# The input rows of the expert tiles turned by the DMA in 16-bit halves instead of on TensorE

## The reference

```python
attn_out = attention(q, kv, w_sr)       # 2 x 12288 queries of 128, 768 pooled keys each
x = attn_out.reshape(24576, 128)
x = moe(x, w_gate, w1, w2)              # expert = argmax(x @ w_gate), 8 experts, F = 1024
                                        # out = gate * (relu(x @ w1[e]) @ w2[e])
x = moe2(x, w_gate, w_output_gate, w1, w2)   # the same, times sigmoid(x @ w_output_gate)[e]
```

## Time and profile before

| | us |
|---|---|
| median of 3 runs | 1875.81 (1872.98 to 1877.0) |
| profiled execution, span from first to last instruction | 2009.7 |
| PE busy | 1918.1 (95%) |
| PEld busy | 1879.5 (94%) |
| DVE busy | 1342.6 (67%) |
| ACT busy | 1054.8 (52%) |
| POOL busy | 739.4 (37%) |
| `turn_x` on PE (L1287), 400 transposes, busy | 76.3 |

### The profile page before, as it was taken

One profiled execution on the slowest core, in us unless ns is written; L12 is line 12 of the kernel. 1 busy time (PEld: TensorE's weight loads), 2 busy tenths in 40 slices (PEclk: granted clock), 3 DMA queues, 4 the chain that ended last, 5 costly groups with the idle time before them and its releaser, 6 DMA issues. The chain is left out here.

```text
span 2009.7 us, 53289 instructions
## 1 busy us (share of the span) xinstructions
PE 1918.1 (95%) x15716; PEld 1879.5 (94%) x15716; DVE 1342.6 (67%) x3525; ACT 1054.8 (52%) x2333; POOL 739.4 (37%) x823
## 2 busy tenths in 40 slices
PE   9999999999999999998999989899999999999998
PEld 7999999999999989898898889888999999999998
DVE  6788887888887666565566666666655555555555
ACT  3777777777776344344344444343444444444444
POOL 5456643466643323222222222222333333333333
PEclk8999999999999999999999999999999999999999
DMA  8355532355533211111321111142211114141111
GB/s 301 104 169 174 178 102 74 109 172 175 173 114 125 67 49 50 42 46 44 118 92 44 45 48 42 51 135 74 66 44 46 43 42 165 42 163 43 46 44 36
DMA packets 138040, 185.88 MB, mean 92 GB/s; under 512 B 17425, under 2 KB 95380, under 8 KB 134368
## 3 DMA queue, kind: packets, MB, share of 16 engines
q1 hardware_dynamic: 112640, 134.16, 20.9%
q0 software_dynamic: 25312, 50.65, 7.1%
HBM read 98.41 MB, written 87.63 MB: 93 GB/s over the span
## 5 line engine op out<-in xcount | busy, mean ns | idle before, releaser
L1718 DVE SCALAR_TENSOR_TENSOR h_lo<-psum,h_hi 128x512 fp32r<-128x512 f32 x800 | 541.2, 688 | 248.3 <-ACT h_hi L1509 198.4
L1509 ACT ACTIVATE h_hi<-psum 128x512 fp32r<-128x512 f32 x800 | 460.6, 598 | 259.1 <-PE psum L1303 244.9
L1303 PE MATMUL psum<-x_hi,w 128*128 128x256 f32 x1600 | 344.7, 290 | 66.6 <-DVE x_lo L1712 48.7
L413 POOL DMA_INDIRECT y_bucket<-kv_store,place x200 | 194.3, 971 | 542.1 <-DVE place L379 484.5
L1303 PE MATMUL psum<-x_hi,w_split 128*128 128x256 f32 x1600 | 339.6, 287 | 9.2 <-issue 2.8
L997 POOL DMA_INDIRECT out<-rows x200 | 193.9, 970 | 405.0 <-DVE rows L1738 368.5
L1303 PEld LDWEIGHTS psum<-x_hi,w 128*128 128x128 f32 x1600 | 270.2, 192 | 75.5 <-issue 55.2
L1320 PE MATMUL psum<-h_hi,w 128*128 128x256 f32 x1600 | 321.6, 285 | 0.7 <-DVE h_lo L1718 0.7
L413 POOL DMA_INDIRECT x_bucket<-rows,place x192 | 190.0, 990 | 293.2 <-DVE place L379 197.7
L1303 PEld LDWEIGHTS psum<-x_hi,w_split 128*128 128x128 f32 x1600 | 265.5, 189 | 17.4 <-issue 10.5
L1320 PEld LDWEIGHTS psum<-h_hi,w 128*128 128x128 f32 x1600 | 266.4, 195 | 1.3 <-DVE h_lo L1718 1.3
(11 more groups left out here) (177 smaller groups left out, 4385.1 us busy)
## 6 DMA issues: line engine op xcount, KB each, us to landing
w_table<-w_split SPq DMA_DIRECT2D x64, 512.0 KB, 3.5
w_raw<-in_moe_w SPq DMA_DIRECT2D x64, 256.0 KB, 4.1
xr<-x_bucket SPq DMA_DIRECT2D x100, 132.0 KB
xr<-y_bucket SPq DMA_DIRECT2D x100, 132.0 KB
kv_store<-in_kv SPq DMA_DIRECT2D x24, 512.0 KB, 9.3
q_in<-in_q SPq DMA_DIRECT2D x48, 256.0 KB, 2.7
w<-w_table SPq DMA_DIRECT2D x12, 1024.0 KB, 6.8
w_split<-w_table SPq DMA_DIRECT2D x8, 1024.0 KB
```

The lines of the kernel that those rows point to most:

```text
L413: nc.gpsimd.indirect_dma_start(r.bucket[:, :], bass.IndirectOffsetOnAxis(r.place[:, g, s:s + 1], 0), r.rows[:, g, s, LG:], None, bounds_ch ...
L1303: ins = nc.tensor.matmul(bank[p][:, m * BLOCK:(m + 1) * BLOCK], layer.w1[c % 2][:, hl, f], x[:, c % 2, :], start=k == 0, stop=k == 2)
L1509: nc.scalar.activation(h_hi[:, p, :], bank[p][:, :], ACT.Relu).then_inc(h_hi_done, 1)
L1718: nc.vector.scalar_tensor_tensor(h_lo[:, p, :], bank[p][:, :], 0.0, h_hi[:, p, :].bitcast(F32), ALU.max, ALU.subtract).then_inc(h_lo_done, 1)
```

## The change

Rows are stored in the tables with their 16-bit halves parted: 128 low halves, then 128 high halves. GpSimd does that in a new step `halve`, a copy of 128x512 elements of 16 bits for each half group (each block or tile), out of a new tile `pre_rows` (`pre_mid` in layer 1) into `rows`. `load_x` becomes two DMAs: a transposing one of 256 rows by 256 halves into `x_halves`, and a small one for `ID` and `GATE` into `tags`. VectorE gets a new step `join_x` at the front of each tile (ahead of `h_low` 0), a copy of 128x512 elements of 16 bits that puts the halves together again to float32 in `x_whole` (a part of `w_raw`). `x_high` and `x_low` read `x_whole` in SBUF instead of PSUM bank 5; `turn_x` is gone from TensorE. Row t of a tile is now token t of the load, where it was (2p + s); both sides of the row, the matmul and `tags`, follow that.

```diff
-PITCH = 132
+PITCH = 130
...
+        x_halves = sb("x_halves", [P, 4, 2, BLOCK], U16)
+        tags = sb("tags", [P, 4, SUB, PITCH - D], I32)
+        x_whole = w_raw[:, 0, 0:2 * BLOCK].rearrange("p (k t) -> p k t", k=2)
...
+        def halve(pool, r, i, gc):
+            if live(i, gc, r.groups, 2):
+                g = gc % 2
+                for h in range(2):
+                    at = slice(h * SUB, (h + 1) * SUB)
+                    wait(pool, r.row_step, i, UNROLL * r.row_steps, r.row_steps * (2 * gc + h + 1))
+                    pool.sem_inc(r.halve_go, 1)
+                    pool.tensor_copy(r.rows[:, g, at, 0:D].bitcast(U16).rearrange("p s (k d) -> p s k d", k=2),
+                                     r.pre[:, g, at, r.n * E:r.n * E + D].bitcast(U16)
+                                     .rearrange("p s (d k) -> p s k d", k=2)).then_inc(r.halved, 1)
+
         def scatter(pool, r, i, gc, h):
...
+                wait(pool, r.halved, i, 4, 2 * gc + h + 1)
                 pool.sem_inc(r.scatter_go, 1)
...
-                def load_x(i, c, layer):
+                def load_x(i, c, layer, k):
...
-                    return sp.dma_start(xr[:, c % 4],
-                                        layer.r.bucket[bass.ds(row, BLOCK), 0:PITCH].rearrange("(p s) c -> p s c", s=SUB))
+                    sp.dma_start_transpose(x_halves[:, c % 4],
+                                           layer.r.bucket[bass.ds(row, BLOCK), 0:D].bitcast(U16)).then_inc(x_in[k], 16)
+                    sp.dma_start(tags[:, c % 4], layer.r.bucket[bass.ds(row, BLOCK), D:PITCH]
+                                 .rearrange("(s p) c -> p s c", p=P)).then_inc(tags_in[k], 16)
...
                     pool.tensor_tensor(rid, rid, id_step[:, :], ALU.add).then_inc(ids_done, 1)
+                    halve(pool, r1, i, gc)
                     wait(pool, ids_done, i, 2, gc + 1)
                     scatter(pool, r1, i, gc, 0)
...
                 with pool.Fori(0, TIT - 2) as i:
                     for gc in range(2):
+                        halve(pool, r2, i, gc)
                         for h in range(2):
                             scatter(pool, r2, i, gc, h)
...
-                def turn_x(i, c):
-                    if tile_live(i, c):
-                        if at(i, c, 0):
-                            pe.wait_ge(p_lo_done, PAIRS * (NBLK - 1) + 2)
-                        wait(pe, x_in[c % 4], i, 16, 16 * (c // 4 + 1))
-                        wait(pe, x_lo_done, i, UNROLL, c)
-                        for s in range(SUB):
-                            ins = nc.tensor.transpose(bank[5][:, s * P:(s + 1) * P], xr[:, c % 4, s, 0:D], ident[:, :])
-                        ins.then_inc(x_turned, 1)
...
                         tile_rows(i, c - 1, n)
-                        turn_x(i, c + 1)
                         up(i, c, 3, n)
...
-                        nc.scalar.activation(rows[:, g, h:h + SUB, LG - E:LG + C], rows_ps(1), ACT.Copy) \
+                        nc.scalar.activation(pre_rows[:, g, h:h + SUB], rows_ps(1), ACT.Copy) \
                             .then_inc(r1.row_step, 1)
...
-                        wait(act, x_turned, i, UNROLL, c + 1)
+                        wait(act, x_joined, i, UNROLL, c + 1)
                         wait(act, up_done, i, HP * UNROLL, HP * (c - 1))
-                        nc.scalar.activation(x_hi[:, c % 2, :], bank[5][:, 0:BLOCK], ACT.Copy).then_inc(x_hi_done, 1)
+                        nc.scalar.activation(x_hi[:, c % 2, :], x_whole[:, c % 2, :], ACT.Copy).then_inc(x_hi_done, 1)
...
+                def join_x(i, c):
+                    if tile_live(i, c):
+                        if at(i, c, 0):
+                            dve.wait_ge(split_done[1], 2 * NPART * E)
+                        wait(dve, x_in[c % 4], i, 16, 16 * (c // 4 + 1))
+                        wait(dve, x_lo_done, i, UNROLL, c - 1)
+                        nc.vector.tensor_copy(x_whole[:, c % 2, :].bitcast(U16).rearrange("p (t k) -> p k t", k=2),
+                                              x_halves[:, c % 4]).then_inc(x_joined, 1)
...
-                        nc.vector.tensor_tensor(x_lo[:, c % 2, :], bank[5][:, 0:BLOCK],
+                        nc.vector.tensor_tensor(x_lo[:, c % 2, :], x_whole[:, c % 2, :],
                                                 x_hi[:, c % 2, :].bitcast(F32), ALU.subtract).then_inc(x_lo_done, 1)
...
+                        wait(dve, tags_in[c % 4], i, 16, 16 * (c // 4 + 1))
+                        nc.vector.tensor_copy(to[:, g, h:h + SUB, ID],
+                                              tags[:, c % 4, :, ID - D]).then_inc(row_step, 1)
+                        nc.vector.tensor_tensor(into, rows_ps(2)[:, :, skip:],
+                                                bcast(tags[:, c % 4, :, GATE - D].bitcast(F32), 2 * E + D - skip), ALU.mult) \
                             .then_inc(row_step, 1)
...
+                        join_x(i, c + 1)
                         h_low(i, c, 0)
```

More of the change, by code:

```diff
@@ L29 @@
 I32 = mybir.dt.int32
+U16 = mybir.dt.uint16
 ALU = mybir.AluOpType
@@ L155, in moe_kernel @@
         oT = sb("oT", [P, 2, BLOCK])
-        rows = sb("rows", [P, 2, GSUB, LG + LINE])
+        rows = sb("rows", [P, 2, GSUB, LINE], I32)
+        pre_rows = sb("pre_rows", [P, 2, GSUB, E + C])
         before = sb("before", [P, P], BF16)
@@ L307, in route @@
             ns = len(r.steps)
-            logits = r.rows[:, g, :, LG - r.n * E:LG - r.n * E + E]
+            logits = r.pre[:, g, :, 0:E]
             def after(step):
@@ L371, in route @@
                 after("den")
-                nc.vector.reciprocal(r.rows[:, g, :, LG + GATE], den_g[:, 2])
+                nc.vector.reciprocal(r.rows[:, g, :, GATE].bitcast(F32), den_g[:, 2])
             elif name == "placed":
@@ L413, in scatter @@
                     nc.gpsimd.indirect_dma_start(
-                        r.bucket[:, :], bass.IndirectOffsetOnAxis(r.place[:, g, s:s + 1], 0), r.rows[:, g, s, LG:], None,
+                        r.bucket[:, :], bass.IndirectOffsetOnAxis(r.place[:, g, s:s + 1], 0), r.rows[:, g, s, :], None,
                         bounds_check=E * STRIDE - 1, oob_is_err=False).then_inc(r.scattered[g][h], 16)
@@ L633, in moe_kernel @@
         x_in = [sem(f"x_in{k}") for k in range(4)]
-        x_turned = sem("x_turned")
+        tags_in = [sem(f"tags_in{k}") for k in range(4)]
+        x_joined = sem("x_joined")
         x_hi_done = sem("x_hi_done")
@@ L981, in _ @@
                 with pool.Else():
+                    pool.wait_ge(r2.halved, 4 * (TIT - 2))
+                    pool.sem_inc(r2.halved, 4)
                     for gc in range(2):
+                        halve(pool, r2, TIT - 1, gc)
                         for h in range(2):
@@ L997, in scatter_out @@
                         nc.gpsimd.indirect_dma_start(
-                            out[:, :], bass.IndirectOffsetOnAxis(rows[:, g, s, LG + ID:LG + ID + 1].bitcast(I32), 0),
-                            rows[:, g, s, LG:LG + D], None, bounds_check=N - 1, oob_is_err=False) \
+                            out[:, :], bass.IndirectOffsetOnAxis(rows[:, g, s, ID:ID + 1], 0),
+                            rows[:, g, s, 0:D].bitcast(F32), None, bounds_check=N - 1, oob_is_err=False) \
                             .then_inc(out_done[g], 16)
@@ L1727, in tile_rows_out @@
                         if layer.n == 1:
-                            to, skip = r2.rows, 0
+                            to, into, skip = r2.rows, r2.pre[:, g, h:h + SUB], 0
                             if not at(i, c, TILES - 1):
```

61 lines of the change are left out of this document (29 added, 32 removed).

## The result

| | us |
|---|---|
| changed kernel, median of 4 runs | 1847.54 (1844.63 to 1850.2) |
| kernel before beside it, median of 4 runs | 1876.40 (1872.98 to 1877.58) |
| ratio | 0.9853, 95% interval 0.9841 to 0.9866 |
| profiled execution of the changed kernel: its own time, its span | 1850.2, 1848.3 |

The change made the kernel 28.9 us faster, 1.5%. The forecast was 55 us faster: the sign was right, the size twice too large.

The account below looks back on a forecast made before the run. TensorE was taken as the bound in both layers. Turns 33 us plus late cases 24 us, added work 0, made 57 us of the 2009.7 us span, giving 1821 us; range 1790 to 1880.

Parts of the forecast that it names:

- Layer 1's 48 late cases: TensorE's up 0 in layer 1 waits for x_lo; x ready earlier gains 0.5 us a case, 24 us (bounds 0.3 to 1.0).
- The turns: Two transposes of x less per tile on TensorE: 0.22 us in each of 152 tiles, 33 us.
- The added half: Join on VectorE, halves on GpSimd, transposing DMA and moved sources: all off TensorE's path or covered, 0 us.
- x's window of 5.7 us: Time from SP's issue of x to its join; with h_lo 0's cover a landing up to 7.4 us is free.
- The term of 3 us: Landing time taken for x's transposing DMA, between bounds 2.2 and 9.3 us, at 0 cost.
- The estimate of 5.2 us: Transposing DMA's time if its four 128x128 blocks go one after the other at 1309 ns; barely within the window.
- Rival C: Transposing DMA lands too late, from 7.4 us on, and the join holds h_lo 0; 2000 us at 9.3; chance 0.13.
- SP's issue: SP has time for a longer issue and a second DMA for x, each 0.55 us; no cost.
- Rival A: Layer 1's idle time on TensorE stays, only the other 152 tiles gain 33 us: 1845 us; chance 0.18.
- B: GpSimd becomes late in attention: 16-bit copies of 2.6 us cost 57 us, cancelling the gain: 1876 us; chance 0.07.
- D: Join runs in several passes or blocks GpSimd's descriptors; h_lo late in layer 1, 20 us back, 1840 us; chance 0.07.
- signs: No L1287 on TensorE, layer 2 tiles 0.22 us shorter, layer 1 idle time at down 2 under 67 us.

Follow-up runs that it names:

- the turns alone: Kernel before with its 400 transposes of x left out: 1873.24 us against 2012.63 (ratio 0.9304) on a 2000 chip, 1837.48 (0.9805) on a 1875 chip.

## Why the prediction came out twice too large

**Layer 1's 48 late cases, 24 us: the step that failed.** On a chip as fast as that of the result there are none: 3.2 us of waits in the kernel before instead of 67.3, and none of them for x_lo. The rows were read rightly, of another chip. The warning stood in the prediction, "the median of the runs is 133.9 us less than the span", and I answered it with a factor of 0.97, which assumes a difference spread over everything. The earlier trace rows held an idle time of 67 us with a slower clock behind it: I should have asked whether the shorter median is just this trace without its stalls. With the earlier trace rows it can be checked: 99 tiles of layer 1 took 728.8 us in that trace and 627.2 on a 1875 chip, 101.6 of the 133.9. For the kind of chip that the trace showed, the term was too small instead (93 us measured for the whole, 57 forecast, and 139 for the turns alone): a stall costs more than its idle time, since the matmuls behind it are slow, and most of a case comes back. With these cases gone the sum had 33 us left; the two terms below moved it by +4.7 and -9.7.

**The turns, 33 us for 152 tiles.** All 200 count where there are no stalls; 43.6 us of slots. 37.7 came, since layer 2's matmuls went 1.2% slower without the turns; the layer 2 tiles were to be 0.22 us shorter and got 0.13 shorter. The trace of before has such slow matmuls too, but nothing in it tells that on another chip they would come with the change.

**The added half, 0 us.** 5.6 us in the traces, 9.7 by the medians. The halves were sized well and the join was shorter than its 0.65 us, but their cover ends at one place I had not looked at: tile 0 behind the attention, 2.2 us, where join, x_hi and x_lo stand in line and GpSimd's halves hold VectorE. Waits for weights, 5.9 us against 3.1 without turns, take most of the rest. Sum: 37.7 - 9.7 = 28.0 by the medians of one chip, 28.9 in the result.

**x's window of 5.7 us** held: the join starts 5.4 us (median) behind the issue, with six waits in 200, and 56 us of waits when a second transposing DMA stood in front. The term of 3 us was right, 2.8 measured. The estimate of 5.2 us that the prediction worked out from the Trainium skill's figure (page "VectorE: DVE Perf Modes", section "The three transpose paths") did not come: four blocks in one DMA took 2.8 us. Rival C did not come, but one more such DMA costs 22 us. SP's issue was mis-sized, 1.22 us instead of 0.55; no run shows a cost of that.

**Rival A** gave 1845, and 1847.5 came: that is luck, its number by a false mechanism. It let the idle time stay; there was none. Rivals B and D did not happen. What I named as signs held: no L1287, no wait for x_lo in layer 1, and on the 2000 chip the idle time at `down`, released by h_lo, 31 us.

## What to carry to other kernels

When the profiled span and the unprofiled median differ by more than a per cent or two, first ask which stage could hold the difference, and value the gains in it twice, with and without its stalls; a common factor hides exactly that. A link in a chain between engines has two prices, its slot and its latency, and on a machine that reports late the second can be larger: moving two transposes by half a tile was worth 111 us there and -6 elsewhere, so a change of order is to be timed on more than one chip.

## What the runs showed of the hardware

- One kernel, one core: 1875 us on two of the chips with a known number and 1995 to 2013 on three, all executions of it on one chip within 1.0%. Three quarters of the difference are in layer 1 (7.37 us a tile against 6.34), where ScalarE starts on TensorE's results 2.5 to 3.0 us late in the two cases shown, around the time of the scatters.
- On 1875 chips matmuls of 256 columns start 113.3 ns apart in layer 2 with four transposes a tile, and with two transposes 117.5 ns apart for a third of them, at a granted clock of 1.00 in either stretch. On a 2000 chip the slow kind is there with four as well (415 of 1419 distances). Cause unknown.
- A 256x256 transposing DMA of 16-bit elements holds SP 1.22 us at the issue and lands 2.8 us after its start (median), against 2.6 for a plain load of as many bytes. 197 more of them brought the packets from 246842 to 354010, 544 each; the median landing of a 1 MB load was 6.0 to 6.6 us without such DMAs, 7.0 with one a tile and 6.4 with two.
- A copy of 128x512 16-bit elements with a stride of two takes 0.45 us on VectorE, 0.61 to 0.64 on GpSimd.
